# Choosing TensorE's slot size by a tree, once per slot, and adding matmuls on constants to the routing

## The chip, the cores and the metric

One Trainium2 chip, one of its cores. The metric is the device time of one launch in microseconds (us).

## The reference, cut to what matters

Three stages follow one another. First attention with a window: 4 batches, 8 heads, 576 positions, head size 64. Its output is 2304 tokens (rows) of 512 numbers, `x`. Then a mixture of experts with one expert per token, and then a dense two-layer network with softplus:

```
logits = x @ w_gate;  e_idx = argmax(logits)            # 8 experts
gate_w = softmax(logits)[e_idx];  eom = sigmoid(x @ w_output_gate)[e_idx]
out[tokens of e] = gate_w * eom * (relu(x @ w1[e]) @ w2[e])      # 512 -> 1024 -> 512
h = out @ w_in;  result = softplus(h) @ w_out                    # 512 -> 2048 -> 512
```

## The kernel before, in words

**Routing.** After attention, VectorE works out the expert of every token, its rank among the tokens of that expert, and from these where each token goes, in a chain of small instructions. Each runs through `step` (it increments the semaphore `route_step` and VectorE waits for it), which makes them numbered steps. TensorE takes part four times: L573 and L574 (rank and count of tokens, bfloat16 products on the one-hot matrix), L578 (18 products that give which token sits in each row of each block of 128 rows), L583 (18 products that give each row's scale), and L593 (12 transposes of the first slot's rows, 4 for each of 3 blocks). L578 and L583 read their moving operand with a stride of 36 bytes. Between them GpSimd gathers the first slot's rows (L420) by the indices that VectorE copies out of L578's result, and VectorE multiplies them by the row scales (`scale_first`, L1102) after L583. VectorE also clears four accumulation banks (`zero_y`, L1082) between L583 and the transposes.

**Slots.** Tokens are sorted by expert into slots of up to 384 rows. There are 8 slots and up to 5 more for experts with over 384 tokens. For a slot TensorE does 8 hidden chunks of 128, as 2 halves of 4 (`half_slot_products`). A chunk has a first product (L614 to L616, 12 matmuls into `h_ps`) and a second product (L627 to L629, 12 matmuls into `yT_ps`); each half also has 6 transposes of the next slot's rows (L600). Three matmuls stand for one because every number is held as a high and a low part. ScalarE makes the high parts (w_hi L812, h_hi L827, x_parts L831), VectorE the low parts (w_lo L1070, h_lo L1088, x_parts L1078), and SyncE loads the weights.

**Choice of the size.** The instructions of a half exist six times over in TensorE's program, once for each of 384, 352, 320, 288, 256 and 224 rows. `slot_products` loads the number of rows taken (L674) and then, in each half, goes down a chain: is it over 352, over 320, over 288, and so on. At each level of the chain there are two branches, L681 (if over) and L683 (if not). The loop over the two halves is L686 and stands outside the chain. Its other queues (ScalarE, VectorE, GpSimd, SyncE) don't choose a size: they always handle 384 rows.

**Last network.** L614 to L616 and L636 to L640 do six groups of 384 rows, with fixed sizes and no branches inside.

The order of the work is written out by hand for each engine, and engines meet at semaphores.

Of the kernel before, what the change touches and what calls it, by code (L numbers as in the profile page):

```python
# [71 lines left out]
def build(nc, qT, kT, vw, wg, we, wm, out):  # L72
    assert OVER == 5 and NT * P == N and GROUPS * SLOT == N
    ctx = ExitStack()
    with ctx:
# [116 lines left out]
        rank_ps, tot_ps, source_ps, scale_ps = bank[1], bank[2], bank[3], bank[4]  # L192
# [283 lines left out]
        def _(pe):  # L476
# [93 lines left out]

            pe.wait_ge(onehot_ready, 1)
# [3 lines left out]

            pe.wait_ge(block_tokens, 2)
# [3 lines left out]
            last.then_inc(sources_summed, 1)  # L580
            pe.wait_ge(block_scales, 1)
# [6 lines left out]
            def first_transposes():  # L588
                pe.wait_ge(row_scales_ready, 1)
                for j in range(TPS):  # L590
                    pe.wait_ge(first_scaled, j + 1)
                    for k in range(KC):
                        last = nc.tensor.transpose(first_t_ps[k][:, P * j:P * (j + 1)],  # L593
                                                   first_xs[:, j, P * k:P * (k + 1)], ident[:, :])
                        if j == TPS - 1:
                            last.then_inc(rows_t_done, 1)

# [75 lines left out]
            def slot_products(slot):  # L673
# [3 lines left out]
                def from_size(half, n):  # L677
                    if n == len(SIZES) - 1:
                        half_slot_products(slot, half, parity, SIZES[n])
                        return  # L680
                    with pe.If(taken > SIZES[n + 1]):  # L681
                        half_slot_products(slot, half, parity, SIZES[n])
                    with pe.If(taken <= SIZES[n + 1]):  # L683
                        from_size(half, n + 1)

                with pe.Fori(0, HALF) as half:  # L686
                    from_size(half, 0)
# [212 lines left out]
        def _(dve):  # L900
# [147 lines left out]
            step(V.reciprocal(R["scale"][:, :], R["den"][:, :]))  # L1048
            dve.wait_ge(sources_summed, 1)
# [7 lines left out]
            step(V.tensor_copy(scale_piece[:, 0, :], R["scale"][:, :]))  # L1057
            step(V.tensor_tensor(R["rest"][:, :], R["scale"][:, :], scale_piece[:, 0, :], ALU.subtract))
            step(V.tensor_copy(scale_piece[:, 1, :], R["rest"][:, :]))
            step(V.tensor_tensor(R["rest"][:, :], R["rest"][:, :], scale_piece[:, 1, :], ALU.subtract))  # L1060
            step(V.tensor_copy(scale_piece[:, 2, :], R["rest"][:, :]))
# [19 lines left out]
            def zero_y(k):  # L1081
                nc.vector.memset(yT_ps[k][:, 0:SLOT], 0.0).then_inc(y_zeroed, 1)  # L1082
# [27 lines left out]
            step(V.tensor_scalar(SL["expert8"][:, :], SL["expert"][:, :], float(-E), None, ALU.add))  # L1110
            dve.wait_ge(scales_summed, 1)
# [5 lines left out]
            scale_first(0)  # L1117
            for k in range(KC):
                zero_y(k)
# [4 lines left out]
            scale_first(1)  # L1124
# [111 lines left out]
```

## Time and profile before

| | us |
|---|---|
| three runs | 852.86, 854.55, 854.78 (median 854.55) |
| the profiled execution, its own time | 856.93 |
| its span, first to last instruction | 855.17 |
| TensorE (PE) busy | 782.6 (92%) |
| VectorE (DVE) busy | 445.3 (52%) |
| ScalarE (ACT) busy | 399.4 (47%) |
| GpSimd (POOL) busy | 216.4 (25%) |
| mean granted TensorE clock, 1.00 being 2.4 GHz | 0.958 |

All times below count from the start of the span. PE's busy time includes matmuls that run at half clock, and its idle time before an instruction is put down to what released it. "issue" means that the profile shows nothing that the instruction waited for. Register and branch instructions are not counted as busy, and show up only where a line is asked for; there PEldq is TensorE's sequencer.

### The profile page before, as it was taken

The page shows a single profiled execution, that of the slowest core. Times are in us where ns is not written, and L with a number is a line of the kernel's source. Part 1 is how long each engine was busy: PE and PEld are TensorE (multiplying, and loading weights), DVE is VectorE, ACT ScalarE, POOL GpSimd, SP SyncE. Part 2 cuts the span into 40 slices and gives each one's busy share as a digit, 9 for nine tenths or more (in the row PEclk, how much of TensorE's full clock was granted, in tenths as well). Part 3 has the DMA queues.
Part 4 walks back from the last instruction along what each step waited for, and adds up shares of the span by engine and source line. Part 5 has one row for each costly group of instructions (what it writes and reads, how often), then busy time and mean ns, then how long its engine had stood idle before and what let it go on. Part 6 is the DMA issues. An engine that isn't in the chain of part 4 may idle for free.

```text
span 855.2 us, 14148 instructions
## 1 busy us (share of the span) xinstructions
PE 782.6 (92%) x4658; PEld 703.4 (82%) x4659; DVE 445.3 (52%) x905; ACT 399.4 (47%) x1014; POOL 216.4 (25%) x218
## 2 busy tenths in 40 slices
PE   5998994688799999789979999999999999999996
PEld 3676673478799989789979989999999999999995
DVE  8876976734354557567556343334334334334332
ACT  3985973123354545455446344334335335335332
POOL 6220220722434465456572001001001001001001
PEclk9999997598899999999989999999999999999999
DMA  9678102454444555565440000000000000000000
GB/s 243 165 186 303 54 0 110 135 174 133 129 133 163 172 165 175 186 194 160 137 126 22 1 1 37 0 0 37 0 0 37 0 0 37 0 0 37 0 0 37
DMA packets 27262, 74.62 MB, mean 87 GB/s; under 512 B 4112, under 2 KB 12320, under 8 KB 26720
## 3 DMA queue, kind: packets, MB, share of 16 engines
q1 hardware_dynamic: 20624, 53.52, 20.4%
q0 software_dynamic: 5744, 16.02, 6.1%
q10 hardware_dynamic: 864, 4.72, 1.4%
q8 instruction: 15, 0.25, 0.1%
q14 instruction: 15, 0.12, 0.0%
HBM read 64.79 MB, written 9.45 MB: 87 GB/s over the span
## 4 chain that ended last, share of the span: by engine, by line
PE 85%; DVE 6%; issue 3%; ACT 2%; DMA 1%; SPq 1%; POOL 0%; DVEq 0%; ACTq 0%
PE bank L614 13%; PE bank L615 12%; PE bank L616 12%; PE bank L638 8%; PE bank L640 8%; PE bank L636 8%; PE bank L494 4%; PE bank L627 4%; PE bank L629 4%; PE bank L628 4%; PE bank L518 2%; PE bank L531 2%; PE bank L504 2%; DVE w_lo L1070 2%; DMA v_sb<-vw 1%
## 5 line engine op out<-in xcount | busy, mean ns | idle before, releaser
L1183 DVE SCALAR_TENSOR_TENSOR g_sb<-bank,soft 128x384 f32<-128x384 f32 x96 | 53.6, 558 | 235.7 <-ACT soft L880 235.7
L876 ACT ACTIVATE soft<-bank 128x384 f32<-128x384 f32 x96 | 47.3, 492 | 209.4 <-PE bank L616 209.4
L614 PE MATMUL bank<-x_parts,w_hi 128*128 (+1 forms) x352 | 118.0, 335 | 26.3 <-issue 19.4
L1070 DVE TENSOR_TENSOR w_lo<-raw,w_hi 128x1024 fp32r<-128x1024 f32 x68 | 95.4, 1404 | 64.5 <-ACT w_hi L812 64.3
L615 PE MATMUL bank<-x_parts,w_hi 128*128 (+1 forms) x352 | 116.3, 330 | 0.0
L616 PE MATMUL bank<-x_parts,w_lo 128*128 (+1 forms) x352 | 116.2, 330 | 0.0
L466 POOL DMA_INDIRECT out<-y_sb,out_rows_i x18 | 17.5, 972 | 379.0 <-ACT y_sb L887 375.3
L812 ACT ACTIVATE w_hi<-raw 128x1024 fp32r<-128x1024 f32 x68 | 71.7, 1058 | 58.3 <-PE bank L629 57.5
L614 PEld LDWEIGHTS bank<-x_parts,w_hi 128*128 128x128 f32 x352 | 72.5, 206 | 30.6 <-issue 29.5
L627 PE MATMUL bank<-h_hi,w_hi 128*128 128x384 f32 (+3 forms) x256 | 81.0, 317 | 2.5 <-DVE h_lo L1088 2.5
L401 POOL TENSOR_SCALAR xs_sb<-landing,row_scale 128x256 f32<-128x256 f32 x48 | 47.7, 1001 | 121.0 <-PE bank L600 120.9
L749 ACT ACTIVATE probs<-bank,neg_max 96x128 f32<-96x128 f32 x192 | 67.3, 364 | 23.0 <-DVE neg_max L919 23.0
L629 PE MATMUL bank<-h_lo,w_hi 128*128 128x384 f32 (+3 forms) x256 | 77.6, 303 | 0.0
L628 PE MATMUL bank<-h_hi,w_lo 128*128 128x384 f32 (+3 forms) x256 | 77.5, 303 | 0.0
L615 PEld LDWEIGHTS bank<-x_parts,w_hi 128*128 128x128 f32 x352 | 72.3, 205 | 1.0
L616 PEld LDWEIGHTS bank<-x_parts,w_lo 128*128 128x128 f32 x352 | 72.1, 205 | 0.0
L827 ACT ACTIVATE h_hi<-bank 128x384 fp32r<-128x384 f32 x64 | 31.5, 493 | 86.4 <-PE bank L616 86.2
L614 PE MATMUL bank<-x_parts,m_hi 128*128 128x384 f32 x192 | 65.6, 342 | 5.3 <-DVE x_parts L1169 5.3
L616 PE MATMUL bank<-x_parts,m_lo 128*128 128x384 f32 x192 | 65.4, 341 | 0.0
L615 PE MATMUL bank<-x_parts,m_hi 128*128 128x384 f32 x192 | 65.3, 340 | 0.0
L1088 DVE SCALAR_TENSOR_TENSOR h_lo<-bank,h_hi 128x384 fp32r<-128x384 f32 x64 | 35.4, 554 | 50.3 <-ACT h_hi L827 50.3
L640 PE MATMUL bank<-m_hi,h_lo 128*128 128x512 f32 x144 | 57.0, 396 | 0.0
(197 smaller groups left out, 1796.8 us busy)
## 6 DMA issues: line engine op xcount, KB each, us to landing
raw<-we SPq DMA_DIRECT2D x64, 512.0 KB, 3.3
x_tokens<-x_sb ACTq DMA_DIRECT2D x6, 768.0 KB, 5.1
v_sb<-vw SPq DMA_DIRECT2D x4, 1024.0 KB, 13.5
raw_m<-wm POOLq DMA_DIRECT2D x8, 512.0 KB, 4.7
raw<-wm SPq DMA_DIRECT2D x8, 512.0 KB, 3.3
q_sb<-qT SPq DMA_DIRECT2D x4, 768.0 KB, 9.0
k_sb<-kT SPq DMA_DIRECT2D x8, 384.0 KB, 11.6
v_sb<-vw SPq DMA_DIRECT2D x4, 512.0 KB, 5.0
```

Of the source, the lines that this page charges most:

```text
L614: nc.tensor.matmul(bank_[:, 0:rows], hi[:, w], x_part(0, k), start=(k == 0), stop=False)
L615: nc.tensor.matmul(bank_[:, 0:rows], hi[:, w], x_part(1, k), start=False, stop=False)
L616: last = nc.tensor.matmul(bank_[:, 0:rows], lo[:, w], x_part(0, k), start=False, stop=(k == KC - 1))
L627: nc.tensor.matmul(y, hi[:, w], h_hi[:, h, 0:rows], start=False, stop=False, skip_group_check=True)
L628: nc.tensor.matmul(y, lo[:, w], h_hi[:, h, 0:rows], start=False, stop=False, skip_group_check=True)
L629: last = nc.tensor.matmul(y, hi[:, w], h_lo[:, h, 0:rows], start=False, stop=(i == RING - 1), skip_group_check=True)
L636: nc.tensor.matmul(y_ps[j][:, :], h_hi[:, f % HRING, c], hi[:, DM:2 * DM], start=(f == 0), stop=False, skip_group_check=True)
L638: nc.tensor.matmul(y_ps[j][:, :], h_hi[:, f % HRING, c], lo[:, DM:2 * DM], start=False, stop=False, skip_group_check=True)
L640: last = nc.tensor.matmul(y_ps[j][:, :], h_lo[:, f % HRING, c], hi[:, DM:2 * DM], start=False, stop=(f == FC2 - 1), skip_group_check=True)
L749: last = nc.scalar.activation(probs[:, c, h, :], s_ps[c][0:QT, KEYS * h:KEYS * (h + 1)], ACT.Exp, bias=neg_max[:, c, h:h + 1], scale=SCALE ...
L812: nc.scalar.activation(w_hi[:, r, :], raw[:, r, :], ACT.Copy).then_inc(done, 1)
L1070: nc.vector.tensor_tensor(w_lo[:, r, :], raw[:, r, :], w_hi[:, r, :].bitcast(F32), ALU.subtract).then_inc(w_lo_done, 1)
```

## The change: what it does

Four edits.

1. `slot_products` asks for the size once per slot, by a tree: over 288, then over 352 or over 256, and so on. The loop over the two halves now stands inside each of the six copies.
2. `keep_running(n)` issues n matmuls of 128x128 by 128 columns in bfloat16 on constants, into columns that nobody reads. `keep_pace` issues three after each of VectorE's steps 1 to 6, 9 to 24, 35 to 37 and 38 to 50, which is 38 times; `first_transposes` adds 8 after each of its three blocks.
3. VectorE's five steps that split the scale into three bfloat16 pieces move ahead of its wait for L578; its clearing of the four banks moves ahead of its wait for L583, which is possible as `scale_ps` moves from bank 4 to bank 3.
4. The three `scale_first` stand together, after the step chain that gives the slots' sizes. `first_transposes` no longer waits for `row_scales_ready`.

```diff
-        rank_ps, tot_ps, source_ps, scale_ps = bank[1], bank[2], bank[3], bank[4]
+        rank_ps, tot_ps, source_ps, scale_ps = bank[1], bank[2], bank[3][:, 0:P], bank[3][:, P:2 * P]
...
+            def keep_running(n, bank_=bank[0]):
+                for _ in range(n):
+                    nc.tensor.matmul(bank_[:, SLOT:SLOT + P], ones_b[:, :], lower_b[:, :], start=True, stop=True,
+                                     skip_group_check=True)
+
+            def keep_pace(steps):
+                for value in steps:
+                    pe.wait_ge(route_step, value)
+                    keep_running(3)
+
+            keep_pace(range(1, 7))
             pe.wait_ge(onehot_ready, 1)
...
+            keep_pace(range(9, 25))
             pe.wait_ge(block_tokens, 2)
...
+            keep_pace(range(35, 38))
             pe.wait_ge(block_scales, 1)
...
             def first_transposes():
-                pe.wait_ge(row_scales_ready, 1)
+                keep_pace(range(38, 51))
                 for j in range(TPS):
                     pe.wait_ge(first_scaled, j + 1)
...
+                    keep_running(8, bank[0] if j < TPS - 1 else bank[7])
...
-                def from_size(half, n):
-                    if n == len(SIZES) - 1:
-                        half_slot_products(slot, half, parity, SIZES[n])
+                def of_size(sizes):
+                    if len(sizes) == 1:
+                        with pe.Fori(0, HALF) as half:
+                            half_slot_products(slot, half, parity, sizes[0])
                         return
-                    with pe.If(taken > SIZES[n + 1]):
-                        half_slot_products(slot, half, parity, SIZES[n])
-                    with pe.If(taken <= SIZES[n + 1]):
-                        from_size(half, n + 1)
-
-                with pe.Fori(0, HALF) as half:
-                    from_size(half, 0)
+                    middle = len(sizes) // 2
+                    with pe.If(taken > sizes[middle]):
+                        of_size(sizes[:middle])
+                    with pe.If(taken <= sizes[middle]):
+                        of_size(sizes[middle:])
+
+                of_size(SIZES)
...
             step(V.reciprocal(R["scale"][:, :], R["den"][:, :]))
+            step(V.tensor_copy(scale_piece[:, 0, :], R["scale"][:, :]))
...
             dve.wait_ge(sources_summed, 1)
...
-            step(V.tensor_copy(scale_piece[:, 0, :], R["scale"][:, :]))
...
+            for k in range(KC):
+                zero_y(k)
             dve.wait_ge(scales_summed, 1)
...
             dve.wait_ge(row_scales_ready, 1)
-            scale_first(0)
-            for k in range(KC):
-                zero_y(k)
...
-            scale_first(1)
...
-            scale_first(2)
+            for j in range(TPS):
+                scale_first(j)
```

## Rows read from the trace of the kernel before

**Rows 1.** Windows by stage: routing, slots, last network (length, busy per engine, PEclk granted)
```profile
134.45:165.46 31.01, 11.33 (x51) 7.22 (x51) 23.49 (x74) 5.49 (x11) 12.46 (x12) 0.57 0.28 84
165.46:439.50 274.04, 246.99 (x1632) 242.25 (x1632) 154.53 (x207) 122.83 (x188) 136.29 (x120) 0.94 0.51 162
444.83:855.17 410.34, 403.55 (x2016) 366.00 (x2016) 158.25 (x316) 170.92 (x332) 25.72 (x25) 0.99 0.03 13
```

**Rows 2.** Waits of PE in the slots (us in total, times, longest us)
```profile
PE bank L614 <- issue: 19.4, 8, 5.1
```

**Rows 3.** Timeline of PE, first matmul after each longer idle time (start us, us)
```profile
188.91 0.44 PE L614 MATMUL bank<-x_parts,w_hi 128*128 x1 [2.43 <-issue]
...
211.77 0.60 PE L614 MATMUL bank<-x_parts,w_hi 128*128 x1 [3.69 <-issue]
...
233.04 0.60 PE L614 MATMUL bank<-x_parts,w_hi 128*128 x1 [5.13 <-issue]
...
316.55 0.55 PE L614 MATMUL bank<-x_parts,w_hi 128*128 x1 [2.06 <-issue]
...
331.37 0.36 PE L614 MATMUL bank<-x_parts,w_hi 128*128 x1 [1.48 <-DVE w_lo L1070]
...
347.18 0.55 PE L614 MATMUL bank<-x_parts,w_hi 128*128 x1 [2.83 <-issue]
...
377.17 0.39 PE L614 MATMUL bank<-x_parts,w_hi 128*128 x1 [2.17 <-issue]
...
392.74 0.39 PE L614 MATMUL bank<-x_parts,w_hi 128*128 x1 [0.44 <-issue]
...
408.23 0.41 PE L614 MATMUL bank<-x_parts,w_hi 128*128 x1 [1.80 <-DVE w_lo L1070]
```

**Rows 4.** Branch lines on TensorE's sequencer, whole run, then window 344:347.3 (ns min/median/max)
```profile
L681 PEldq COMPARE_BRANCH  x52: 68/208/3005, 164.8 to 423.7; - x52
L683 PEldq COMPARE_BRANCH  x52: 67/72/4746, 183.2 to 436.9; - x52
...
L681 PEldq COMPARE_BRANCH  x5: 210/210/214, 344.6 to 346.3; - x5
L683 PEldq COMPARE_BRANCH  x5: 67/67/67, 344.9 to 346.5; - x5
```

**Rows 5.** Windows after three restarts: length, PE busy (matmuls), PEclk, DMA share, GB/s
```profile
211.77:218.77 7.00, 7.00 (x33) 0.59 0.33 107
...
316.55:320.55 4.00, 4.00 (x21) 0.58 0.79 222
331.37:335.37 4.00, 4.00 (x34) 1.00 0.64 208
```

**Rows 6.** Lines L578 and L583, TensorE (ns min/median/max, first and last start)
```profile
L578 PE MATMUL bank<-block_token,place_onehot x18: 332/334/355, 145.8 to 148.5; 128*128 128x84 bf16 x18
L583 PE MATMUL bank<-block_scale,place_onehot x18: 404/410/428, 152.2 to 156.2; 128*128 128x126 bf16 x18
```

**Rows 7.** Timeline of the routing, PE (start us, us)
```profile
138.02 0.42 PE L573 MATMUL bank<-onehot_b,lower_b 128*128 128x144 bf16 x1 [3.56 <-DVE onehot_b L1000]
138.25 0.44 PE L574 MATMUL bank<-onehot_b,ones_b 128*128 128x144 bf16 x1
...
162.56 1.11 PE L593 MATMUL bank<-ident,first_xs 128*128 128x128 f32 x4 [0.57 <-DVE first_xs L1102]
...
165.46 0.68 PE L614 MATMUL bank<-x_parts,w_hi 128*128 x1 [1.78 <-DVE x_parts L1078]
...
173.03 0.44 PE L627 MATMUL bank<-h_hi,w_hi 128*128 128x384 f32 x1 [1.20 <-DVE h_lo L1088]
```

**Rows 8.** Timeline of the routing, DVE (start us, us)
```profile
149.77 0.17 DVE L1057 CAST scale_piece<-route_scale 128x18 bf16<-128x18 f32 x1
...
150.83 1.34 DVE L1062 TENSOR_TENSOR block_scale<-in_block,scale_piece 128x2268 bf16<-128x2268 bf16 x1
...
157.94 1.60 DVE L1082 MEMSET bank<- 128x384 f32 x4
```

More of the change, by code:

```diff
@@ L1048, in _ @@
             step(V.reciprocal(R["scale"][:, :], R["den"][:, :]))
+            step(V.tensor_copy(scale_piece[:, 0, :], R["scale"][:, :]))
+            step(V.tensor_tensor(R["rest"][:, :], R["scale"][:, :], scale_piece[:, 0, :], ALU.subtract))
+            step(V.tensor_copy(scale_piece[:, 1, :], R["rest"][:, :]))
+            step(V.tensor_tensor(R["rest"][:, :], R["rest"][:, :], scale_piece[:, 1, :], ALU.subtract))
+            step(V.tensor_copy(scale_piece[:, 2, :], R["rest"][:, :]))
             dve.wait_ge(sources_summed, 1)
@@ L1056, in _ @@
                             ).then_inc(half_sources_ready, 1)
-            step(V.tensor_copy(scale_piece[:, 0, :], R["scale"][:, :]))
[L1058 to L1061, printed above, removed]
             V.tensor_tensor(block_scale[:, :, :, :],
```

## The prediction

> **What bounds the kernel now.** I read the windows by stage first [rows 1]. In the slots PE is busy 247.0 of 274.0 us and in the last network 403.6 of 410.3; no other engine passes 57%. In the routing PE is busy 11.3 of 31.0 us, at a granted clock of 0.57, so mostly at 1.2 instead of 2.4 GHz, while DVE is busy 23.5: that stage is DVE's chain with PE's answers in it. The change touches the routing and the slots; the last network I leave as it is.
>
> In the slots 27.1 us are idle. The waits put 19.4 of them, in 8 pieces, on "issue" [rows 2], and the timeline shows the pieces where a half or a slot begins [rows 3]. Two of its entries name w_lo as releaser. I don't believe that: the first product of a half waits for a chunk that the code splits three chunks ahead. They fit the branches. At a start with 224 rows the sequencer goes through five L681 and five L683 between 344.6 and 346.5 [rows 4]: a level that fails costs 0.21 (jump over a copy) and 0.07, with the pauses between them 0.4 us (1.7 us for four spacings). Most branches cost that little, but the longest L681 takes 3.0 and the longest L683 4.7 us. Such a branch must wait for code, and the three longest idle times (2.43, 3.69, 5.13, all before 234 us [rows 3]) are where copies are left or entered for the first time.
>
> Idle time costs twice. After 3.69 us idle the clock is 0.59 for 7 us, in which 33 matmuls ran. After 2.06 us idle, 21 matmuls ran in 4 us at 0.58, and after 1.48 us idle 34 at 1.00 [rows 5]: 13 matmuls of 0.118 us are a loss of 1.5 us. A mean of 0.58 over 4 us is 3.4 us at half clock, 0.59 over 7 us is 5.7, so I price the half clock after a long idle time at 1.5 x 5.7 / 3.4 = 2.5 us.
>
> **The tree, second halves.** The loop's back edge now leads to code that has just run, with no question. Five second halves give back their idle time: slot 0 2.43 + 1.5; slot 1 5.13 + 2.5; the two 224-row slots 2 x 1.48 (one shown, the other alike); slot 6 0.44 [rows 3]. Sum 15.0. Hidden once that is gone: DVE's and ACT's parts for the next chunk; in the 224-row slots these are late next, so 2 x 1.48 could be 2 x 0.8 (bounds of this term 13.6 to 15.0).
>
> **The tree, slot starts.** A level is 0.4 us. Slots 4, 5 and 6 (224, 224, 288 rows) pass two failing levels fewer: 0.8 each, 2.4. Their idle times become 1.3, 2.0 and 1.4. Idle of 2.06 and 1.80 was followed by half clock and 1.48 was not, so slots 4 and 6 keep their clock: 2 x 1.5 = 3.0 (bounds 0 and 3.0). Slots 2 and 3 pay a branch more each on entering or leaving the 384 copy: -0.4. Slot 7 stays.
>
> Slot 1 pays what slot 0's second half no longer does. Leaving copy 384 for the first time, the sequencer jumps to the question "not over 288", three copies further on, and from there to the end of the tree: two places not reached before. Before, the start had one slow branch of 3.0 in its 3.69 us. Now there are two of 3.0 to 4.7, I take 3.9 each: 3.69 - 3.0 - 0.8 + 7.8 = 7.7 us idle, 4.0 worse (bounds 2.2 and 5.6, or a gain of 0.8 if one block of code serves all). The half clock after it stays.
>
> Slots together: 15.0 + 2.4 + 3.0 - 0.4 - 4.0 = 16.0 us.
>
> [...]
>
> **The routing.** DVE's five pieces (149.77 to 150.83 [rows 8]) move into its wait for L578: 1.06 earlier. L578 takes 18 x 0.159 = 2.9 us and L583 18 x 0.235 = 4.2 [rows 6], at half clock. If only the clock set these they would halve (gain 3.6). But per column they take 1.9 ns, and L573 to L574, at full clock, 0.23 us for 144 strided columns [rows 7], so 1.6 ns. I take 1.6: 0.45 + 0.6 = 1.05 us (bounds 0 and 3.6).
>
> [...]
>
> From the end of L583 to the end of L593's last block there are 7.1 us (156.6 to 163.67 [rows 6, 7]). DVE's share shrinks by the 1.6 us of clearing [rows 8], but PE now has 39 matmuls on constants before the transposes and 16 between them. A pair of load and matmul has no row of this shape; it is bounded by 0.053 (128 columns at 2.4 GHz) and 0.23 (L573 to L574). At 0.053 PE keeps DVE's pace and 1.5 are won; at 0.11, which is the same at half clock, it lags and 1.1 are lost. I take 0. The eight behind the last transpose are issued ahead of the slot loop's registers: 0.5 later for the first product, which has room, as will be seen.
>
> The first products then run at full clock and end 2 us sooner, but the second product of slot 0 waits for DVE's h_lo [rows 7]: DVE goes from the split rows through 18 position steps to h_lo, whatever PE does. So it starts only as much earlier as DVE's chain, 1.06 + 1.05 + 0 = 2.1 us, and the idle time of 1.20 ahead of it grows to some 2.7, enough for a half clock after it: -1.5. Routing 0.6 us, bounds -2.9 (every pair slow, L578 unchanged) and +6. The matmuls after steps 1 to 24 lie beside DVE's steps of 0.2 to 0.5 us; without that cover each set of three would delay rank or source products by under 0.3. No DMA is moved; GpSimd's gathers start with L578's result, and the queues of SP and POOL keep their order.
>
> **Sum.** 16.0 + 0.6 = 16.6 us from the profiled execution's 856.93 (span 855.17 and 1.8 around it): 840.3. That execution was 2.4 above the median of 854.55, so for the median I take the same 16.6 off: 838.0. A difference under 0.3%, 2.6 us, can't be told from none.
>
> **The rivals.**
> 1. A third slow branch remains (0.22). The 4.7 us L683 at the end of slot 1's first half led to the loop's end, which slot 0 had already reached at 183 us. If blocks of code are dropped like that, leaving slot 1 stalls again: 3.9 and 2.5 of clock are 6.4 us less gain: 844.4.
> 2. The constants do all that they can (0.18): clock full from step 9, L578 and L583 halved, PE at pace, no half clock after h_lo. Routing then gives 6 instead of 0.6: 832.6. For it speaks that PE is empty otherwise at 0.57 clock; against it the 1.6 ns per column.
> 3. Slower (0.04): jumps of the tree miss again and again, because the tree jumps further (three copies) than the chain (one) and TensorE's program is longer by some 280 instructions. Two slow branches at each of the 6 later slot starts, 12 x 3.9 = 47 us, less the 16.6: 885. It decides from the fifth repeated miss on (16.6 / 3.9 = 4.3). Against it: no idle time of the slots after 234 us is over 2.83 us now. [...]
> 4. The tree's code for slot 1 comes with one slow branch (0.10): 3.9 better, 834.1.
> 5. The constants do nothing, or hold PE up (0.08): the clock of the routing stays, PE lags DVE; routing -2.9 instead of 0.6: 841.5. That is the case in which that part of the change doesn't do what it says.
>
> The forecast itself has 0.38. Cases 1, 2, 4 and 5 and the bounds of the terms (13.6 for the second halves; clock of slots 4 and 6 worth 0; slot 1 -5.6) make the range 829.5 to 848. Faster 0.94, same 0.02, slower 0.04.
>
> **What would show it.** Right: L614 has no idle time over 0.5 us at second halves; L683 or L681 show two entries over 3 us, both near 200 us; idle at the starts of slots 4 and 6 under 1.5 with clock 1.00 after it; the "if over" branches passed 20 times instead of 52 (by the sizes of the eight slots). Wrong: slow branches after slot 1; L578 spacing at 0.08 us; slot 0's second product starting much before 170.9; a last network of other than 410 us.

## The result, and the profile after

The changed kernel takes **843.79 us** (median of 4 runs, 843.16 to 844.76), the kernel before 854.15 in the same measurement (4 runs, 852.86 to 854.78): a ratio of 0.9882, with an interval of 0.9864 to 0.9899. The forecast was 838.0 in a range of 829.5 to 848, so the sign and the range hold, and the gain is 10.4 us where 16.6 were forecast. A repeat of the same kernel, below, gave 845.36 and 0.9916 [0.9888, 0.9944]. Both are nearest to the first rival, a third slow branch, which was worked out at 844.4.

The page of the changed kernel: span, the engines' busy time, TensorE's granted clock in 40 slices, and the shares of the chain that ended last.

```profile
span 842.2 us, 14340 instructions
...
PE 783.4 (93%) x4796; PEld 705.6 (84%) x4797; DVE 440.8 (52%) x905; ACT 398.9 (47%) x1014; POOL 222.5 (26%) x218
...
PEclk9999998799889999999989999999999999999999
...
PE 86%; DVE 7%; issue 4%; ACT 2%; POOL 0%; DVEq 0%; ACTq 0%
```

The stages, as windows (columns as in [rows 1]): routing, slots, last network.

```profile
134.45:163.55 29.10, 22.96 (x188) 18.43 (x189) 22.64 (x73) 5.06 (x10) 11.18 (x10) 0.71 0.29 95
163.55:427.02 263.47, 236.60 (x1632) 233.49 (x1632) 149.58 (x207) 122.57 (x188) 144.07 (x122) 0.96 0.51 167
432.36:842.20 409.84, 403.00 (x2016) 365.68 (x2016) 158.25 (x316) 170.76 (x332) 25.48 (x25) 0.99 0.03 13
```

The span is 13.0 us shorter (855.17 to 842.20); that is more than the 10.4 us of the medians, as the execution profiled before was 2.4 over its median. The routing has PE busy for 23.0 instead of 11.3 us (188 matmuls instead of 51, the new ones on constants) and a clock of 0.71 instead of 0.57, and yet it is only 1.9 us shorter. The slots hold the surprise. PE's idle time in them is 263.47 - 236.60 = 26.9 us, and before it was 274.04 - 246.99 = 27.1 [rows 1]: **nothing of the idle time went away**. What fell is busy time, by 10.4 us for the same 1632 matmuls, so they ran at a better clock (0.96 in the window instead of 0.94). Not all of that is the change's doing: routing_only below has the chain of before, and its slots have 3 us less busy time than those of the kernel before, too (from slot 0's second product on 240.6 us before, 237.5 in routing_only, 232.1 in the changed kernel). The idle time only moved. The waits of PE in the slots say where to (us in total, times, longest):

```profile
PE bank L628 <- issue: 18.8, 4, 10.1
PE bank L641 <- DVE h_lo L1103: 5.0, 3, 3.4
PE bank L628 <- DVE w_lo L1085: 3.0, 3, 1.4
```

It is 18.8 us in 4 pieces on "issue" instead of 19.4 in 8 [rows 2]. The pieces, from PE's timeline (start us, us, and in brackets the idle time before it):

```profile
171.45 0.44 PE L641 MATMUL bank<-h_hi,w_hi 128*128 128x384 f32 x1 [3.44 <-DVE h_lo L1103]
...
212.30 0.60 PE L628 MATMUL bank<-x_parts,w_hi 128*128 x1 [10.06 <-issue]
...
246.96 0.69 PE L628 MATMUL bank<-x_parts,w_hi 128*128 x1 [5.48 <-issue]
...
315.42 0.37 PE L628 MATMUL bank<-x_parts,w_hi 128*128 x1 [1.16 <-DVE w_lo L1085]
...
341.76 0.37 PE L628 MATMUL bank<-x_parts,w_hi 128*128 x1 [1.94 <-issue]
...
367.49 0.50 PE L628 MATMUL bank<-x_parts,w_hi 128*128 x1 [1.33 <-issue]
```

L628 and L641 are the L614 and L627 of before. No second half has a longer idle time ahead of its first product any more, and the starts of slots 4 to 6 are shorter by 0.8 to 0.9 each. But slot 1 waits 10.06 instead of 3.69 us, and slot 2 waits 5.48, where the kernel before had no long wait at all [rows 3] (0.65 us). The branch lines on TensorE's sequencer tell why (ns min/median/max, first and last start; whole slots, then two short windows):

```profile
L697 PEldq COMPARE_BRANCH  x20: 65/206/232, 162.6 to 396.2; - x20
L699 PEldq COMPARE_BRANCH  x20: 67/72/5984, 199.2 to 424.7; - x20
...
L699 PEldq COMPARE_BRANCH  x2: 4259/5122/5984, 199.2 to 203.5; - x2
...
L699 PEldq COMPARE_BRANCH  x1: 4751/4751/4751, 239.6 to 239.6; - x1
```

20 passes instead of 52, as worked out. Three are slow: 4.3 and 6.0 us one after the other when copy 384 is left for the first time (199.2 and 203.5), and 4.8 us when slot 1's copy is left (239.6). Before there were three too, of 4.4, 3.0 and 4.7 us. So the tree removed no waiting for code: it asks less than half the questions, and the three that wait take 15.0 us instead of 12.2.

That these branches wait for code can be read from the DMA queues. The profile has a queue q8 that it calls "instruction", with packets of 16 KB. Its rows (packets, MB, share), for the slots of the changed kernel, for 199 to 210 and for 239 to 247 us in it, and for the slots of the kernel with four sizes (experiment 4):

```profile
q8 instruction: 8, 0.13, 0.2%
...
q8 instruction: 3, 0.05, 1.8%
...
q8 instruction: 2, 0.03, 1.7%
...
q8 instruction: 4, 0.07, 0.1%
```

The same for every profiled execution: the branches of TensorE over 1 us from the routing to the end of the slots (in us from the start of the span), with the packets of q8 that start inside them, and the number of its packets in the slots:

```
run               branches over 1 us: start, us (starts of the q8 packets inside)     packets in the slots
changed kernel    199.2 4.26 (201.1); 203.5 5.98 (205.4, 206.8); 239.6 4.75 (242.1)   8
kernel before     183.2 4.40 (185.2); 207.9 3.00 (208.5); 225.8 4.75 (228.2)          8
tree_only         201.5 4.10 (203.2); 205.6 6.13 (207.2, 209.0); 241.7 4.71 (244.1)   8
routing_only      183.3 4.49 (185.3); 208.0 2.92 (208.6); 223.3 5.00 (226.0)          8
no_constants      198.8 4.44 (200.8); 203.3 6.03 (205.3, 205.6); 239.9 4.69 (242.2)   8
four_sizes        200.7 5.47 (202.1, 202.1)                                           4
after_again       200.1 4.14 (201.8); 204.3 5.96 (205.6, 207.2); 240.4 4.65 (242.8)   8
chain_once        203.2 4.19 (205.0); 210.0 5.21 (212.8); 242.6 5.00 (245.3)          8
fill              198.1 4.80 (200.2); 203.0 5.95 (204.7, 204.7); 239.0 4.73 (241.4)   8
touch             138.9 3.39 (139.9); 202.8 5.57 (204.2, 204.5)                       4
fill_four         197.7 5.63 (199.2, 199.2)                                           4
fill_three        196.3 4.06 (198.0)                                                  3
fill_four_again   196.2 5.48 (197.6, 198.0)                                           4
four_sizes_again  204.1 6.02 (205.7, 205.8)                                           4
```

These are 31 branches in 14 profiled executions, and every one of them has a packet of q8 starting inside it. The 21 with one packet take 2.9 to 5.2 us, the 10 with two take 5.5 to 6.1. The slots of the kernel before have 8 packets as well. Not every packet falls into such a branch: in the changed kernel four of the eight do, and the others start at 165.1, 210.2, 215.6 and 245.5 us. From 247 to 440 us there is none here, and from 247 us to the end of the slots no branch takes over 0.23 us.

The routing on PE:

```profile
137.37 0.42 PE L584 MATMUL bank<-onehot_b,lower_b 128*128 128x144 bf16 x1
...
138.63 4.38 PE L573 MATMUL bank<-lower_b,ones_b 128*128 128x128 bf16 x45 [0.58 <-DVE cum L1026]
...
145.17 3.00 PE L590 MATMUL bank<-block_token,place_onehot 128*128 128x84 bf16 x18 [0.64 <-DVE block_token L1053]
...
150.55 4.34 PE L596 MATMUL bank<-block_scale,place_onehot 128*128 128x126 bf16 x18 [0.87 <-DVE block_scale L1077]
154.71 4.34 PE L573 MATMUL bank<-lower_b,ones_b 128*128 128x128 bf16 x39
...
161.34 0.61 PE L573 MATMUL bank<-lower_b,ones_b 128*128 128x128 bf16 x8
```

L590 and L596 (the L578 and L583 of before) take 3.00 and 4.34 us, as long as before to within 0.1 [rows 6]. The 39 constants take 4.34 us, 0.11 each, at half clock (0.50), which lasts until 159.4 us; the eight that start at 161.34, at full clock, lie 0.056 us apart. The constants hold VectorE up: its parts of the first slot's rows (x_parts, which need the transposes) wait 2.03 us, where they wait 0.94 in the kernel without constants (experiment 3). First the changed kernel, then that one:

```profile
161.73 1.95 DVE L1093 TENSOR_TENSOR x_parts<-bank,x_parts 128x384 fp32r<-128x384 f32 x4 [2.03 <-ACT x_parts L862]
...
160.70 1.95 DVE L1090 TENSOR_TENSOR x_parts<-bank,x_parts 128x384 fp32r<-128x384 f32 x4 [0.94 <-ACT x_parts L859]
```

### The profile page after: what moved, and what is told of

It is laid out like the page before. It is cut to its first block, busy times and chain, and to the rows that moved or that the text cites. A ratio compares the mean times of both kernels' runs of the same rounds, so it can differ in the third digit from the quotient of the medians.

```text
span 842.2 us, 14340 instructions
## 1 busy us (share of the span) xinstructions
PE 783.4 (93%) x4796; PEld 705.6 (84%) x4797; DVE 440.8 (52%) x905; ACT 398.9 (47%) x1014; POOL 222.5 (26%) x218
## 4 chain that ended last, share of the span: by engine, by line
PE 86%; DVE 7%; issue 4%; ACT 2%; POOL 0%; DVEq 0%; ACTq 0%
PE bank L628 13%; PE bank L630 12%; PE bank L629 12%; PE bank L652 8%; PE bank L654 8%; PE bank L650 8%; PE bank L641 4%; PE bank L643 4%; PE bank L642 4%; PE bank L494 3%; PE bank L518 2%; PE bank L531 2%; PE bank L504 2%; DVE w_lo L1085 1%; PE bank L614 1%
## 5 line engine op out<-in xcount | busy, mean ns | idle before, releaser
L628 PE MATMUL bank<-x_parts,w_hi 128*128 (+1 forms) x352 | 113.6, 323 | 23.5 <-issue 18.8
L1085 DVE TENSOR_TENSOR w_lo<-raw,w_hi 128x1024 fp32r<-128x1024 f32 x68 | 89.9, 1324 | 67.6 <-ACT w_hi L827 67.6
L629 PE MATMUL bank<-x_parts,w_hi 128*128 (+1 forms) x352 | 112.7, 320 | 0.0
L630 PE MATMUL bank<-x_parts,w_lo 128*128 (+1 forms) x352 | 112.5, 320 | 0.0
L628 PEld LDWEIGHTS bank<-x_parts,w_hi 128*128 128x128 f32 x352 | 68.8, 195 | 26.4 <-issue 25.3
L641 PE MATMUL bank<-h_hi,w_hi 128*128 128x384 f32 (+3 forms) x256 | 81.2, 317 | 5.0 <-DVE h_lo L1103 5.0
L764 ACT ACTIVATE probs<-bank,neg_max 96x128 f32<-96x128 f32 x192 | 67.3, 365 | 22.6 <-DVE neg_max L934 22.6
L401 POOL TENSOR_SCALAR xs_sb<-landing,row_scale 128x256 f32<-128x256 f32 x48 | 50.1, 1052 | 104.1 <-PE bank L614 104.0
L628 PE MATMUL bank<-x_parts,m_hi 128*128 128x384 f32 x192 | 65.5, 341 | 5.3 <-DVE x_parts L1183 5.3
L629 PEld LDWEIGHTS bank<-x_parts,w_hi 128*128 128x128 f32 x352 | 68.8, 195 | 1.0
L630 PEld LDWEIGHTS bank<-x_parts,w_lo 128*128 128x128 f32 x352 | 68.8, 195 | 0.0
L388 POOL DMA_INDIRECT landing<-x_tokens,half_source_i x48 | 54.3, 1130 | 14.2 <-issue 10.3
```

What stands on the lines that cost most here:

```text
L628: nc.tensor.matmul(bank_[:, 0:rows], hi[:, w], x_part(0, k), start=(k == 0), stop=False)
L629: nc.tensor.matmul(bank_[:, 0:rows], hi[:, w], x_part(1, k), start=False, stop=False)
L630: last = nc.tensor.matmul(bank_[:, 0:rows], lo[:, w], x_part(0, k), start=False, stop=(k == KC - 1))
L641: nc.tensor.matmul(y, hi[:, w], h_hi[:, h, 0:rows], start=False, stop=False, skip_group_check=True)
L764: last = nc.scalar.activation(probs[:, c, h, :], s_ps[c][0:QT, KEYS * h:KEYS * (h + 1)], ACT.Exp, bias=neg_max[:, c, h:h + 1], scale=SCALE ...
L1085: nc.vector.tensor_tensor(w_lo[:, r, :], raw[:, r, :], w_hi[:, r, :].bitcast(F32), ALU.subtract).then_inc(w_lo_done, 1)
```

## The experiments

There were five measurements; the kernels of one ran on the same chip, beside its own runs of the kernel before. Two columns are worked out from each profiled execution: **routing** is the time from VectorE's one-hot to slot 0's second product, **slots** from there to the end of the last slot's products (the one number is the start of the first L641, the other its distance to the last matmul before the last network). They come from one execution each. How far such numbers scatter is seen in routing_only, whose slots have the same instructions as those of the kernel before and are 3.0 us shorter.

```
run               median  before   ratio (interval)          routing  slots   slow branches (us)
changed kernel    843.79  854.15   0.9882 (0.9864, 0.9899)   34.45    255.58  4.3+6.0, 4.8
kernel before       -       -      -                         35.47    266.47  4.4, 3.0, 4.7
-- second measurement
tree_only         845.78  851.14   0.9926 (0.9902, 0.9950)   35.43    255.14  4.1+6.1, 4.7
routing_only      851.89  851.14   1.0011 (0.9987, 1.0034)   34.47    263.48  4.5, 2.9, 5.0
no_constants      844.96  851.14   0.9907 (0.9874, 0.9941)   34.00    257.47  4.4+6.0, 4.7
four_sizes        831.85  851.14   0.9761 (0.9718, 0.9803)   33.03    243.77  5.5
-- third measurement
after_again       845.36  853.68   0.9916 (0.9888, 0.9944)   34.45    255.53  4.1+6.0, 4.7
chain_once        851.92  853.68   0.9975 (0.9947, 1.0003)   34.59    261.57  4.2+5.2, 5.0
fill              842.47  853.68   0.9865 (0.9840, 0.9891)   31.76    255.94  4.8+5.9, 4.7
touch             834.42  853.68   0.9779 (0.9755, 0.9803)   34.72    242.54  3.4 (routing), 5.6
-- fourth measurement
fill_four         845.47  868.65   0.9735 (0.9708, 0.9761)   31.66    242.03  5.6
fill_three        844.20  868.65   0.9714 (0.9683, 0.9744)   31.48    244.34  4.1
-- fifth measurement
fill_four_again   829.34  851.92   0.9732 (0.9714, 0.9750)   31.12    244.54  5.5
four_sizes_again  831.65  851.92   0.9755 (0.9741, 0.9769)   33.44    246.88  6.0
```

The profiled execution of four_sizes_again took 838.42 us, 6.8 over its median.

**1. The tree alone.** The kernel before, with the new slot code and nothing else of the change:

```diff
-                def from_size(half, n):
...
-                with pe.Fori(0, HALF) as half:
-                    from_size(half, 0)
+                def of_size(sizes):
...
+                of_size(SIZES)
```

> The kernel before with the tree alone (no constants, VectorE's order as before). Theory, the changed kernel's gain is nearly all the tree's: slots from slot 0's second product to their end 256 us instead of 266.5, three slow branches (two leaving copy 384, one leaving slot 1), time 844 to 846. Rival, the routing carries half of the gain: 848 to 851.

It takes 845.78 us, 5.4 less than before on that chip. PE's largest wait in its slots is, in this view, that of the changed kernel (L614 is its first product):

```profile
PE bank L614 <- issue: 18.6, 4, 10.0
```

So the gain of the slots, the long wait at slot 1 and the new one at slot 2 all come with the tree.

**2. The routing edits alone.** The changed kernel with the old chain, asked once in each half:

```diff
-                of_size(SIZES)
+                with pe.Fori(0, HALF) as half:
+                    from_size(half, 0)
```

> The changed kernel with the old chain asked in each half. Theory: only the routing's 1 us is left, and the three slow branches stand where they stood before (end of slot 0's first half, start of slot 1, end of slot 1's first half): 852 to 854. Rival, the constants and the new order give half: 847 to 850.

851.89 us, 1.0011 of before with 1 inside the interval: on the whole this part is worth nothing that could be measured. Its routing is 1.0 us shorter (34.47), its slots have the eight pieces of before, and 3.0 us less than the one profile of before:

```profile
PE bank L628 <- issue: 19.6, 8, 5.3
```

**3. The change without its constants.** The helper is empty, and the wait for the row scales is the plain one of before:

```diff
             def keep_pace(steps):
-                for value in steps:
-                    pe.wait_ge(route_step, value)
-                    keep_running(3)
+                return
...
-                keep_pace(range(38, 51))
+                pe.wait_ge(row_scales_ready, 1)
...
-                    keep_running(8, bank[0] if j < TPS - 1 else bank[7])
```

> The changed kernel without any matmul on constants and without their waits on VectorE's steps; tree and VectorE's new order stay. Theory, the constants bring nothing, as the products L590 and L596 run at half clock with them and slot 0 waits for VectorE's h_lo: within 1 us of the changed kernel, 843 to 845, granted clock low until after 165 us, and the wait for h_lo shorter than 3.4 us. Rival, the constants carry the routing's gain: 845.5 or more.

844.96 us, beside 845.78 for the tree alone on the same chip and 845.36 for the whole change on another: no difference that these runs can tell (0.9874 to 0.9941 against 0.9888 to 0.9944). The window of its routing shows the clock that the constants were to lift (length, PE busy, PEclk, DMA share, GB/s):

```profile
136.20:161.00 24.80, 10.79 (x50) 0.50 0.24 71
```

All at the lower of the two levels, and its routing still takes 34.00 us where that with the constants takes 34.45, in both of its profiled executions. So in this kernel they cost 0.45 us there: they hold VectorE's x_parts up by 1.1 us, and the full clock of the first products after them does not make up for it. What makes the routing of the change shorter than that of before is the order of VectorE's steps, 1.4 us (35.43 in tree_only, 34.00 here).

The products L590 do not profit from the clock either, which is seen where they run partly at either level. In the changed kernel (window, PE busy, weight loads, PEclk):

```profile
145.20:145.70 0.50, 0.50 (x4) 0.47 (x5) 1.00 0.00 0
146.00:148.00 2.00, 2.00 (x14) 1.67 (x12) 0.50 0.00 0
```

And in the run with four sizes (experiment 4), where the granted clock fell later:

```profile
146.10:147.50 1.40, 1.40 (x10) 1.28 (x11) 1.00 0.00 0
147.70:148.70 1.00, 1.00 (x8) 0.92 (x7) 0.50 0.00 0
```

Ten matmuls in 1.40 us at a clock of 1.00 and eight in 1.00 at 0.50: 0.14 and 0.13 us each, alike within the one matmul that a window's edge may cut. By their starts they lie 0.15 to 0.16 us apart on both sides, and the same in tree_only, where all 18 run at half clock (146.5 to 149.2 us). So the clock of the array does not set the pace of this strided matmul of 84 columns. What does was not shown: no run here reads the operand without its stride, and L596 (126 columns, 4.33 to 4.34 us for the 18) ran at half clock in every profiled run.

**4. Four sizes instead of six.** The tree is kept, with a third of its code gone:

```diff
-SIZES = (SLOT, 352, 320, 288, 256, 224)
+SIZES = (SLOT, 320, 288, 224)
```

Copies 352 and 256 are used by no slot of this input (the sizes run are 384, 288, 384, 320, 224, 224, 288, 320), so the same products are computed.

> The changed kernel with copies for 384, 320, 288 and 224 rows only; no slot of this data uses 352 or 256, so every matmul is the same, and the code to jump over is a third shorter. Theory, idle time at the starts of slots 1 and 2 is waiting for code that lies some blocks on: one slow branch fewer than three, idle at slot 1's start 5 to 7 instead of 10.1, time 834 to 840. Rival, a slow branch is paid per new place whatever its distance: three slow branches again, 842 to 843.5 by the cheaper questions alone.

It takes 831.85 us, 0.9761 of before, and is below what was expected. The branch line and the idle times at the starts of slots 1 and 6 (slot 5's is 1.57):

```profile
L699 PEldq COMPARE_BRANCH  x16: 71/142/5469, 200.3 to 412.3; - x16
...
208.96 0.60 PE L628 MATMUL bank<-x_parts,w_hi 128*128 x1 [5.64 <-issue]
...
355.55 0.40 PE L628 MATMUL bank<-x_parts,w_hi 128*128 x1 [1.31 <-issue]
```

One slow branch of 5.5 us is left of three. Two copies fewer to jump over took away both the other first visit at slot 1 and the third slow branch at slot 2, and the slots fetch 4 blocks of code instead of 8. They are 11.8 us shorter than those of the changed kernel: 10.6 of idle time (4.4 at slot 1, some 5 at slot 2), and 1.2 of clock. The changed kernel did not run beside it; no_constants did, and takes 13.1 us more. Its routing is 1.4 us shorter as well (1.0 in the repeat). Most of that is the clock: it is full again at 157.8 us, 2.1 us after L596 ends, where the changed kernel has it 4.5 us after. The 39 constants take 3.40 us instead of 4.34, and VectorE's x_parts wait 0.84 instead of 2.03. Why it comes back sooner there is open. The repeat, on another chip:

> Four copies with the constants and VectorE's order of the changed kernel, beside the one above. Theory: 2 to 3 us slower than with the moved steps. Rival, no difference.

It gave 831.65 us and 0.9755 [0.9741, 0.9769], again with one slow branch, of 6.0 us.

**5. Is it the tree, or the loop's place?** The change moved two things at once: the questions became a tree, and the loop over halves went inside the copies. Here the loop is inside and the chain is kept. It ran beside the changed kernel again:

```diff
-                of_size(SIZES)
+                def from_size(n):
...
+                    with pe.If(taken > SIZES[n + 1]):
+                        with pe.Fori(0, HALF) as half:
+                            half_slot_products(slot, half, parity, SIZES[n])
+                    with pe.If(taken <= SIZES[n + 1]):
+                        from_size(n + 1)
+                from_size(0)
```

> The changed kernel with the old chain asked once per slot and the loop over the halves inside each copy. Theory, the loop's place is what pays and the tree's shape adds 0.4 us a level: after copy 384 the chain has one far jump (to the end) instead of two, and slot 1 then jumps one copy at a time to the copy for 288 rows, whose code has not run; two or three slow branches, time within 3 us of the changed kernel. Rival, the tree's fewer questions matter much: over 3 us slower.

> The changed kernel once more, beside the kernels of this call on one chip. Theory: slow branches at the same three places with the same lengths, since they follow from where the code lies (idle of 10 us at slot 1's start, 5.4 at slot 2's). Rival, they depend on chance in the fetching of code: other places or lengths.

The chain asked once takes 851.92 us, not to be told from the kernel before (0.9975, to 1.0003), and 6.6 more than the changed kernel beside it. Its branch lines, PE's wait and one restart:

```profile
L696 PEldq COMPARE_BRANCH  x26: 77/209/5213, 164.2 to 404.0; - x26
L699 PEldq COMPARE_BRANCH  x26: 72/72/4997, 203.2 to 432.1; - x26
...
PE bank L628 <- issue: 22.7, 6, 10.0
...
345.77:349.77 4.00, 4.00 (x22) 0.59 0.58 129
```

I had held the loop's place to be the larger part, and that is wrong. Against routing_only (slots 263.48, the chain in every half) the loop's place brings 1.9 us, which one profile on each of two chips does not prove, and the tree another 6.0 (261.57 to 255.53, on one chip): 2.5 of idle time and 3.5 of busy time. The loop's place takes the idle time from the second halves, and the slow branches that stood there now stand at the slot starts (at 203.2, 210.0 and 242.6 us). The tree's six questions fewer shorten the starts of the small slots, and with that the clock is kept at slot 5: the chain waits 2.74 us there, and then 22 matmuls run in 4 us, where the changed kernel waits 1.94 and runs 34. The length of the wait is not all of it: at slot 4 the chain kept full clock after 1.99 us (34 matmuls in 4 us, 1.00), and at slot 6 both lost it, after 2.12 and 1.33 (17 at 0.50, 18 at 0.57).

**6. VectorE's waits filled.** If the routing is VectorE's chain, work that nobody waits for yet must move into its waits. Without constants, with the tree, and:

```diff
             step(V.tensor_copy(scale_piece[:, 2, :], R["rest"][:, :]))
+            step(V.tensor_tensor_scan(X["counted"][:, :], ...))
+            step(V.tensor_tensor(X["shift"][:, :], ...))
+            step(V.tensor_tensor(X["shift"][:, :], ...))
             dve.wait_ge(sources_summed, 1)
...
-            for k in range(KC):
-                zero_y(k)
+            (the eight steps from RE["tmp"] to position_i, moved up)
             dve.wait_ge(scales_summed, 1)
...
             split_lo(0, 1)
+            for k in range(KC):
+                zero_y(k)
```

> No constants, tree kept, and VectorE's order changed: three of its position steps stand ahead of its wait for the source products, eight more ahead of its wait for the scale products, and the clearing of the four banks behind the first split of the weights, where it waits for the transposes. Theory, slot 0's second product waits for VectorE's chain up to h_lo: 2 to 3 us earlier from the one-hot matrix to that product (31 to 32 us instead of 34.0), time 842 to 843 against 845.0 without the moves. Rival, PE's or ScalarE's part sets that product: no change.

The routing takes 31.76 us, 2.2 less than without the moves (no_constants, on another chip), as expected, at 842.47 us in all. On VectorE, what stands between its last row scale and slot 0's h_lo:

```profile
157.34 0.27 DVE L1141 TENSOR_TENSOR slot_cmp<-slot_expert,emin 128x104 f32<-128x104 f32 x1
...
164.84 2.34 DVE L1085 TENSOR_TENSOR w_lo<-raw,w_hi 128x1024 fp32r<-128x1024 f32 x2
167.11 0.25 DVE L1162 TENSOR_TENSOR slot_tmp<-slot_cmp,expert_shift 128x104 f32<-128x104 f32 x1
...
169.01 0.56 DVE L1103 SCALAR_TENSOR_TENSOR h_lo<-bank,h_hi 128x384 fp32r<-128x384 f32 x1 [0.81 <-ACT h_hi L839]
```

The position steps no longer stand there, h_lo waits for ScalarE's h_hi and not for VectorE, and PE's second product has no wait over 0.4 us. The changed kernel waits 3.44 us there with TensorE at full clock. So in the changed kernel VectorE, and not the clock of the first products, sets the routing's end. In fill that has turned: PE runs without a pause from its first product at 163.74 to the second at 170.43, and 16 of these 24 matmuls run at half clock, 0.32 us apart instead of 0.17. There a full clock could bring up to 2.3 us (16 x 0.145, an estimate); constants together with the moved steps were not tried.

**7. Code touched beforehand.** If the one slow branch of four_sizes waits for code on a first visit, a jump to that place during the routing, when PE is idle, should pay for it there. All code from the source products to the end of the slots stands in a loop of two passes, of which the first skips it (`SIZES` as in experiment 4):

```diff
+            with pe.Fori(0, 2) as visit:
+                with pe.If(visit > 0):
+                    (source products, scale products, transposes, slots)
             used = overflow_slots(pe)
```

> Copies for four sizes, and everything from the source products to the end of the slot loop stands in a loop of two passes, of which the first skips it all: TensorE jumps to the end of the slot loop and back while it would wait for VectorE. Theory, the last slow branch (5.5 us, on leaving slot 0) is the first visit to that code: it moves to about 138 us, where nothing waits for it, idle at slot 1's start under 1 us, time 825 to 828 against 831.9. Rival, the code is dropped again before slot 0 ends: a second slow branch at the same place and no gain.

The first row is the new branch, the second L699 of before under its new number, the third PE's wait at slot 1:

```profile
L588 PEldq COMPARE_BRANCH  x2: 77/1732/3387, 138.9 to 142.8; - x2
...
L701 PEldq COMPARE_BRANCH  x16: 67/140/5567, 202.3 to 413.2; - x16
...
211.12 0.60 PE L630 MATMUL bank<-x_parts,w_hi 128*128 x1 [5.73 <-issue]
```

The jump during the routing cost 3.4 us and was not all hidden: the constants bunch up behind it, and the source products start 1.1 us later after the one-hot than in four_sizes. The branch at slot 1 is as slow as ever (5.57 us, against 5.47 in four_sizes), with two packets of q8 inside it as in four_sizes. So the idea does not pay: 834.42 us. Why not is less clear. The touched place is the end of the slot loop, the slow jump of slot 0 goes to the end of the tree, a few instructions before it, and whether both lie in one block was not measured. That a place once reached can be fetched again is shown without this run, by the third slow branch of the kernels before and after: the same jump target, reached at the end of slot 0's copy, and a packet of q8 again when slot 1's is left (in the changed kernel at 205.4 and 242.1 us).

**8. Both together, and three sizes.** The changes of experiments 4 and 6 in one kernel (four sizes, no constants, waits filled), and the same with the 288 copy removed (`SIZES = (SLOT, 320, 224)`, so that 288-row slots compute 32 rows that nobody uses):

> The two edits that paid together: copies for 384, 320, 288 and 224 rows, no constants, VectorE's steps in its waits. Theory, they add up: one slow branch at slot 1's start (idle 5 to 6 us), 31.8 us from the one-hot matrix to slot 0's second product, time 829 to 831. Rival, the one gain hides the other (clock or fetching shifts): 832 or more.

> As before with three copies, 384, 320 and 224 rows: the two slots of 288 rows run as 320, which by the spacing of their matmuls (0.135 and 0.147 us) costs 2 x 192 x 0.012 = 4.6 us. Theory, the far jump on leaving slot 0 still meets code that has not run: the slow branch stays and the kernel is 4 to 5 us slower than with four copies. Rival, with the end of the tree this near the fetch ahead covers it: slow branch gone, 0 to 3 us faster.

On this chip the kernel before takes 868.65 us. The two take 845.47 and 844.20, and their intervals overlap (0.9708 to 0.9761, 0.9683 to 0.9744). With three sizes the slow branch is shorter, but stays:

```profile
L685 PEldq COMPARE_BRANCH  x14: 72/76/4064, 196.3 to 410.6; - x14
...
203.17 0.41 PE L614 MATMUL bank<-x_parts,w_hi 128*128 x1 [3.81 <-issue]
```

It has one packet of q8 inside, where that of four sizes has two. 2.0 us of idle time are gained against four sizes, and the slots are 2.3 us longer with the wider products: neither expectation came out, and it settles nothing. On this chip both had 21 us of idle time ahead of the last network instead of 5.3; in fill_four ScalarE stood twice in it, for 8.7 and 9.0 us. To see whether that belongs to the kernel, it ran once more elsewhere:

> Four copies and VectorE's moved steps once more, since on the last chip ScalarE stood still for some 15 us at the end of the slots, which no edit here touches. Theory, that wait belongs to that chip: it is gone, and time is 829 to 831. Rival, it comes from these edits: again 21 us idle ahead of the last network.

829.34 us (827.21 to 830.78), 0.9732 [0.9714, 0.9750], with 5.34 us ahead of the last network. So the stand of ScalarE does not come from these edits. It was seen on that chip alone, where the kernel before is slower by about as much. This version is the best found, 22.6 us under the kernel before beside it. The changed kernel did not run beside it; by the ratios (0.9732 against 0.9882 and 0.9916) it is 1.5 to 1.9% under that too. Its lead over four sizes alone on the same chip is 2.3 us, with intervals that overlap (0.9714 to 0.9750, 0.9741 to 0.9769).

## Why the forecast was right and where it was not

**The second halves** (15.0 us) came out: no idle time ahead of one, and the clock that went with it back (slots 0 and 1: 0.66 in the 4 us from 188.91 and 0.65 in the 7 us from 233.04 before, 1.00 in the 7 us from 182.0 and from 226.5 in the changed kernel).

**The levels of the tree** (2.4) came out: 2.06, 2.83 and 2.17 us became 1.16, 1.94 and 1.33. The questions were passed 20 times, as counted.

**Slot 1** (-4.0): two slow branches, as said, but of 4.3 and 6.0 us where I took 3.9 each. The wait was 10.06 instead of 7.7, so the term was too small by 2.4. Its upper bound of 4.7 each came from the longest single branch of the trace before, and there each slow branch fetched one block. The second of the two here fetches two blocks (205.4 and 206.8 us), and such branches take 5.5 to 6.1 us in every run that has one. Where leaving copy 384 leads was misread too, without harm: two copies, not three, lie between it and the question "not over 288".

**Slot 2** (its half of the -0.4) is the step that failed. It was taken as one branch more on the way out, and it had a slow branch of 4.8 us with 5.48 us of idle time, and half the clock after it (0.50 from 246.96 to 250.96 us). This was the first rival at 0.22, and the evidence for it stood in the text: a place that slot 0 had reached was slow again in slot 1. It was read as a possibility, and with six copies it came every time: in all eight profiles of kernels with six copies the place that leaving copy 384 leads to was slow again when slot 1's copy was left, and in none of the six with four or three. I gave it the lower chance because the chain's many other jumps cost 0.21 us each.

**The clock** was priced by the length of the idle time ahead of it, and that was half right. Slot 4 kept its clock and slot 6 did not. Windows of the changed kernel after four restarts, the idle times before them 3.44, 1.16, 1.94 and 1.33 us (length, PE busy, PEclk, DMA share, GB/s):

```profile
171.45:178.45 7.00, 7.00 (x41) 1.00 0.66 233
315.42:319.42 4.00, 4.00 (x34) 1.00 0.66 213
341.76:345.76 4.00, 4.00 (x34) 1.00 0.49 165
367.49:371.49 4.00, 4.00 (x18) 0.57 0.61 187
```

The longest of them was followed by full clock, the second shortest by half. So the idle time just before does not decide it alone, and my border between 1.48 and 1.80 us was none. The errors went both ways. Not lost: 1.5 us after h_lo, which I had charged; 1.5 to 1.7 each at slots 5 and 7, which I had not counted on (in the kernel before 21 matmuls in the 4 us from slot 5's start and 17 from slot 7's, in the changed one 34 and 27). Lost: 1.5 at slot 6, and some 3 at slot 2.

**The account of the slots.** Of idle time I forecast 7.5 us less (11.0 from the second halves, 2.4 from the levels, against 4.0 at slot 1, 0.4 at slots 2 and 3, and 1.5 ahead of h_lo). Measured: 0.2 less, and the 7.3 missing are slot 1 (2.4), slot 2 (4.6) and h_lo (0.7), within 0.5. Of busy time I forecast 7.5 less (4.0 and 3.0 of clock and some 2 in the first product, against 1.5 after h_lo). Measured: 10.4 less. The sum is 10.6 where it was 15, and it stands almost wholly in matmuls that run at a granted clock of 1.00 instead of 0.50. About 3 us of them are not the tree's: routing_only has them as well, against a profile of before that was 2.4 over its median. So that the sum came within a third of the forecast is partly luck: more clock than was priced stands against idle time that did not go away.

**The routing** (0.6, made of 2.1 less 1.5): measured 1.02 from one-hot to second product. Of its terms, the 1.06 of VectorE's five pieces came out. The 1.05 for L578 and L583 was nothing: I had priced the clock's part from L573 to L574. For L578 the experiments show the same spacing at both levels (0.15 to 0.16 us), and L583 ran at half clock again (4.34 us). The 0 for the stretch behind L583 came out as a number (16.5 us from its end to the second product before, 16.6 now), but the case weighed against it did occur: the constants took 0.11 us each and VectorE waited 1.1 us longer for the transposes than without them. The 1.5 after h_lo did not occur. The missing 1.05 and this 1.5 nearly cancel, so that the routing came near its 0.6 is luck.

**The cases.** The second and the fourth did not occur: L590 did not get shorter, and slot 1 had two slow branches. The fifth (constants do nothing, or hold PE up) is true as a mechanism: no_constants and the whole change cannot be told apart, and PE lags VectorE. It was joined with a price of -3.5, which only its worst bound would have had; they cost 0.45. The third (misses at every slot) was ruled out: of 20 passes of L699, 17 take at most 0.22 us. The tree also jumps over three copies at once, in slots 1, 4, 5 and 6, and none of the 20 passes of L697 took over 232 ns.

**Still open:** why in the changed kernel the jump to the end of the tree is slow on its first and second visit (6.0 us at 203.5, 4.8 at 239.6) and takes at most 0.22 us on each later one. Which block of code stands where was not measured; the packets of q8 show when a block comes and not which. It was also not tried to move that place next to the loop's end.

## What to carry to other kernels

Before counting what a shorter chain of branches saves, list the branches that wait for code, and beside them the packets of the instruction queue: here those branches were 3 of 104 before and 3 of 40 after, fell on first and second visits (2.9 to 6.1 us each), and moved to the next slot's start when the loop around them moved, so that less code (two unused copies removed: 10 to 14 us, by ratios and by medians) was worth more than fewer questions (6 us). An idle engine is no reason to give it matmuls on constants (here they cost 0.45 us): ask which engine's chain ends the stage, whether the matmuls that are to profit depend on the clock at all, and whether the added ones are in the way while the clock is still low. And read busy time beside idle time. The same 1632 matmuls in 236.6 busy microseconds instead of 247.0, at 0.96 instead of 0.94, were a gain of clock, and no view of waits showed it.

## What was unexpected of the hardware

- Each of the 31 branches over 1 us has a 16 KB packet of the instruction queue starting in it. With one packet they took 2.9 to 5.2 us, with two 5.5 to 6.1.
- The slots fetched 8 blocks of code in all eight kernels with six copies, 4 in the five profiled with four copies and 3 in the one with three.
- Code that was reached by a far jump waits again some 36 us later (changed kernel: 6.0 us at 203.5, 4.8 at 239.6), while jumps over three whole copies run in 0.20 to 0.23 us.
- An idle time of 3.44 us left the granted clock at full (1.00 in the 7 us after it), one of 1.33 us did not (0.57 in the 4 us after it).
- Strided matmuls of 84 columns lie 0.15 to 0.16 us apart, at a granted clock of 1.00 as at 0.50 (four_sizes, 10 and 8 of them).
- On one of the chips the kernel before takes 868.65 us, where on the others it takes 851 to 854. The ratios of the same new kernel on it and elsewhere are alike (0.9735 and 0.9732).
